# Five products instead of nine for the narrower segment of a two-batch unit

## What is computed

```python
def _attn_ref(q, k, v):            # (4, 8, 576, 64)
    scores = scale * np.matmul(q, k.transpose(0, 1, 3, 2))
    kth = np.partition(scores, -top_k, axis=-1)[..., -top_k:-top_k + 1]   # top_k = 32
    scores = np.where(scores >= kth, scores, -1000000000.0)
    scores = scores - np.max(scores, axis=-1, keepdims=True)
    attn = np.exp(scores)
    attn = attn / (np.sum(attn, axis=-1, keepdims=True) + 1e-09)
    return np.matmul(attn, v)
def _moe_ref(x, w_in, w_out):      # x (2304, 512), d_ff 2048
    h = x @ w_in
    return (h * (1.0 / (1.0 + np.exp(-h)))) @ w_out
def _moe2_ref(x, w1, w2, w3, w_out):   # d_ff 1024
    return (((x @ w1) * (x @ w2)) @ w3) @ w_out
```

## Time and profile before

| | |
|---|---|
| median of 3 runs | 1142.99 us (1142.81 to 1148.94) |
| the profiled execution | 1149.01 us |
| its span, first to last instruction | 1147.2 us |
| PE busy | 1065.4 us, 93% |
| DVE busy | 926.4 us, 81% |
| ACT busy | 773.1 us, 67% |
| POOL busy | 621.9 us, 54% |
| mean DMA rate | 271 GB/s |

### The profile page before, as it was taken

One profiled execution on the slowest core, in us unless ns is written; L12 is line 12 of the kernel. 1 busy time (PEld: TensorE's weight loads), 2 busy tenths in 40 slices (PEclk: granted clock), 3 DMA queues, 4 the chain that ended last, 5 costly groups with the idle time before them and its releaser, 6 DMA issues.

```text
span 1147.2 us, 24502 instructions
## 1 busy us (share of the span) xinstructions
PE 1065.4 (93%) x7968; PEld 995.4 (87%) x7968; DVE 926.4 (81%) x2042; ACT 773.1 (67%) x1921; POOL 621.9 (54%) x803
## 2 busy tenths in 40 slices
PE   2998478899999999999999999999999999999998
PEld 1554477799999999999999999999999999999997
DVE  5788877798888899998989999889899999991110
ACT  4577767777776677776767777767677777774221
POOL 4566768666664455566645555655455445543211
PEclk9999689999999999999999999999999999999999
DMA  9976769986997599779966996899569947963962
GB/s 283 329 270 240 262 234 311 312 262 217 338 354 263 172 326 357 243 245 355 360 210 217 330 343 199 269 356 352 198 224 321 327 145 259 343 212 120 332 242 92
DMA packets 129053, 310.42 MB, mean 271 GB/s; under 512 B 14240, under 2 KB 43936, under 8 KB 128928
## 3 DMA queue, kind: packets, MB, share of 16 engines
q1 hardware_dynamic: 110112, 275.30, 71.1%
q10 hardware_dynamic: 18816, 33.56, 8.3%
HBM read 263.19 MB, written 45.61 MB: 269 GB/s over the span
## 4 chain that ended last, share of the span: by engine, by line
PE 71%; DMA 10%; POOL 4%; DVE 4%; issue 4%; ACT 4%; ACTq 2%; SPq 1%; POOLq 0%; DVEq 0%
PE ps_x L934 7%; DMA win<-win_split 7%; PE ps_h L1002 6%; PE ps_h L1004 6%; PE ps_h L1003 6%; PE ps_s L905 5%; PE ps_h L964 5%; PE ps_h L965 4%; PE ps_h L966 4%; PE ps_y L986 4%; PE ps_y L988 4%; PE ps_y L987 4%; PE ps_t L920 4%; PE ps_y L1015 3%; PE ps_y L1016 3%
## 5 line engine op out<-in xcount | busy, mean ns | idle before, releaser
L809 DVE MAX8 top<-rest 128x8 f32<-128x576 f32 x432 | 309.8, 746 | 0.0
L620 POOL TENSOR_TENSOR g_lo<-gate,g_hi 128x256 fp32r<-128x256 f32 x216 | 160.0, 741 | 251.2 <-ACT g_hi L777 250.9
L811 DVE MATCH_REPLACE8 rest<-top,rest 128x576 f32<-128x576 f32 x288 | 212.9, 743 | 0.5
L964 PE MATMUL ps_h<-x_hi,win 128*128 128x256 f32 x576 | 167.1, 290 | 10.1 <-DMA win<-win_split 9.9
L1002 PE MATMUL ps_h<-x_hi,w_hi 128*128 128x256 f32 x576 | 166.1, 288 | 5.1 <-DVE x_lo L860 4.4
L608 POOL TENSOR_TENSOR pT<-p_raw,pT 128x640 fp32r<-128x640 f32 x72 | 113.4, 1575 | 102.5 <-ACT pT L737 102.5
L986 PE MATMUL ps_y<-g_hi,wout 128*128 128x256 f32 x576 | 165.8, 288 | 1.7 <-POOL g_lo L620 0.9
L1004 PE MATMUL ps_h<-x_hi,w_lo 128*128 128x256 f32 x576 | 162.7, 282 | 0.0
L1003 PE MATMUL ps_h<-x_lo,w_hi 128*128 128x256 f32 x576 | 162.7, 282 | 0.0
L965 PE MATMUL ps_h<-x_lo,win 128*128 128x256 f32 x576 | 162.5, 282 | 0.0
L966 PE MATMUL ps_h<-x_hi,win 128*128 128x256 f32 x576 | 162.3, 282 | 0.0
(11 more groups left out here) (73 smaller groups left out, 2793.8 us busy)
## 6 DMA issues: line engine op xcount, KB each, us to landing
win<-win_split SPq DMA_DIRECT2D x135, 512.0 KB, 6.3
wout<-wout_split SPq DMA_DIRECT2D x135, 512.0 KB, 4.8
wout<-w_dram SPq DMA_DIRECT2D x72, 512.0 KB, 3.9
v_split<-v_dram SPq DMA_DIRECT2D x64, 320.0 KB, 5.7
k_split<-k_dram SPq DMA_DIRECT2D x64, 288.0 KB, 5.7
v_dram<-v_split SPq DMA_DIRECT2D x32, 320.0 KB, 6.0
k_raw<-kT SPq DMA_DIRECT2D x64, 144.0 KB, 5.3
k_dram<-k_split SPq DMA_DIRECT2D x32, 288.0 KB, 6.8
```

What stands on the lines that cost most here:

```text
L809: nc.vector.max(best[:, 8 * n:8 * n + 8], sc if step == 0 else left).then_inc(topk_step, 1)
L811: nc.vector.match_replace(left, best[:, 8 * n:8 * n + 8], sc if step == 1 else left, BELOW_ALL).then_inc(topk_step, 1)
L964: nc.tensor.matmul(ps_h[:, f % 2, 0:UN], hi, xh, start=(c == 0), stop=False)
```

## The change

`beside(u)` names the narrower segment of a unit of two batches and its columns: segment 0 in unit 2, segment 1 in units 4 and 6. For it PV runs four products whose moving operand is two chunks of `pT` at once, the rounded one c and the remaining one c + 5, into two halves of the bank `ps_x`: columns c0 to c1, and the same 256 columns on. The fifth product is chunk 9 into the first half. XS adds the second half's rows of the rounded values to `x_raw` before its old addition; the second half's rows of the remaining values are not used (before, their product with the remaining probabilities was part of the sum). Since the second half of unit 2 lies where the tail was, `tail_at` puts the tail of that unit at column 384.

```diff
+def beside(u):
+    segs = segments(u)
+    if len(segs) < 2:
+        return None
+    n = 0 if segs[0][2] - segs[0][1] < P else 1
+    return n, segs[n][1], segs[n][2]
+
+def tail_at(u):
+    return UN + P if beside(u) and beside(u)[0] == 0 else UN
...
-        ps_tail = ps_x[0:D, UN:UN + P]
+        ps_halves = ps_x[:, :].rearrange("p (a n) -> p a n", a=2)
...
+        def tail(t):
+            at = tail_at(t // 2 // H)
+            return ps_x[0:D, at:at + P]
...
                 elif kind == "XS":
                     s = op[1]
                     dve.wait_ge(x_copied, s + 1)
                     mine = x_raw[hi_cols(s), (s // 2) % 2, :]
+                    if beside(s // H):
+                        _, c0, c1 = beside(s // H)
+                        part = x_raw[hi_cols(s), (s // 2) % 2, c0:c1]
+                        nc.vector.tensor_tensor(part, ps_x[hi_cols(s), UN + c0:UN + c1], part, ALU.add).then_inc(x_part, 1)
+                        dve.wait_ge(x_part, sum(1 for i in range(s + 1) if beside(i // H)))
                     nc.vector.tensor_tensor(mine, ps_x[lo_cols(s), 0:UN], mine, ALU.add).then_inc(x_summed, 1)
...
+                        if beside(s // H) == (seg, c0, c1):
+                            for c in range(KCH - 1):
+                                nc.tensor.matmul(ps_halves[:, :, c0:c1], v_split[:, e % NV, c, :], pT[:, c:c + KCH + 1:KCH, c0:c1],
+                                                 start=(c == 0), stop=False, skip_group_check=True)
+                            m = nc.tensor.matmul(ps_x[:, c0:c1], v_split[:, e % NV, KCH - 1, :], pT[:, 2 * KCH - 1, c0:c1],
+                                                 start=False, stop=True, skip_group_check=True)
+                            continue
```

More of the change, by code:

```diff
@@ L366, in build @@
         normed, transposed, p_rounded, p_split = sem("normed"), sem("transposed"), sem("p_rounded"), [sem("p_split0"), sem("p_split1")]
-        pv_ready, x_copied, x_summed, x_rounded, x_split = sem("pv_ready"), sem("x_copied"), sem("x_summed"), sem("x_rounded"), sem("x_split")
+        pv_ready, x_copied, x_summed, x_part, x_rounded, x_split = sem("pv_ready"), sem("x_copied"), sem("x_summed"), sem("x_part"), sem("x_rounded"), sem("x_split")
         h_ready, tanh_ready, g_ready, g_rounded, g_split = sem("h_ready"), sem("tanh_ready"), sem("g_ready"), sem("g_rounded"), sem("g_split")
@@ L730, in _ @@
                     if on_vector(t):
-                        nc.scalar.copy(pT[0:D, 2 * KCH - 1, cols], ps_tail)
+                        nc.scalar.copy(pT[0:D, 2 * KCH - 1, cols], tail(t))
                     else:
                         nc.scalar.copy(p_raw[:, lane, 0:KCH - 1], ps_t[:, :, :])
-                        nc.scalar.copy(p_raw[0:D, lane, KCH - 1], ps_tail)
-                        nc.scalar.copy(p_raw[D:P, lane, KCH - 1], ps_tail)
-                    nc.scalar.copy(pT[D:P, KCH - 1, cols], ps_tail)
+                        nc.scalar.copy(p_raw[0:D, lane, KCH - 1], tail(t))
+                        nc.scalar.copy(p_raw[D:P, lane, KCH - 1], tail(t))
+                    nc.scalar.copy(pT[D:P, KCH - 1, cols], tail(t))
                     nc.scalar.copy(pT[:, 0:KCH - 1, cols], ps_t[:, :, :]).then_inc(p_rounded, 1)
@@ L830, in _ @@
                                             ALU.subtract)
-                    nc.vector.tensor_tensor(pT[D:P, 2 * KCH - 1, cols], ps_tail, pT[D:P, KCH - 1, cols].bitcast(F32),
+                    nc.vector.tensor_tensor(pT[D:P, 2 * KCH - 1, cols], tail(t), pT[D:P, KCH - 1, cols].bitcast(F32),
                                             ALU.subtract).then_inc(p_split[t % 2], 1)
@@ L920, in _ @@
                         nc.tensor.transpose(ps_t[:, c, :], probs[:, t % 4, P * c:P * c + P], ident[:, :])
-                    nc.tensor.transpose(ps_tail, probs[:, t % 4, P * (KCH - 1):S],
+                    nc.tensor.transpose(tail(t), probs[:, t % 4, P * (KCH - 1):S],
                                         ident[:, :]).then_inc(transposed, 1)
```

## The result

| | before | changed |
|---|---|---|
| median of 20 runs | 1148.76 us | 1141.16 us |
| lowest to highest | 1142.81 to 1156.86 | 1134.75 to 1145.34 |
| profiled execution | 1149.01 | 1139.89 |
| its span | 1147.2 | 1138.0 |

The ratio is 0.9931 with a 95% interval of 0.9913 to 0.9950, that is 7.9 us saved (5.7 to 10.0); 8.3 was forecast. The time itself, 1141.16, lies 0.7 above the range's upper end of 1140.5, because the kernel before takes 1148.76 in the median of 20 runs and not the 1142.99 of the three from which I had subtracted.

The account below looks back on a forecast made before the run. TensorE (PE) was taken to bound all six two-batch stages. Products save 10.2 us, late loads take back 1.9, DVE's addition costs nothing: 8.3 us off the median 1142.99 gives 1134.7 us, range 1131.5 to 1140.5.

Parts of the forecast that it names:

- the base: Whole kernel: the time the saving is taken off, 1142.99 us, median of the runs shown, not the profiled 1149.01.
- The price of a product: PE's value products, 24 two-batch steps: weight load sets the pace, about 0.11 us each; four fewer per step save 10.2 us.
- The two runs of the moving operand: Double products on PE: operand in two runs, five chunks apart, costs nothing; at the dearest column price the sum is 7.2.
- DVE's addition hidden: XS on DVE: 6.6 us added, hidden by DVE's idle time and the 0.96 us before the next transposes.
- DVE at least 6 us busier: Sign in the profile after: DVE's busy time up by this much, with no new wait of the transposes for x_raw.
- What comes late next: First four steps of each two-batch stage: DMA loads of win come late and take back 1.9 us of the gain.
- landing is set by bytes, not by issue: Load of win in a first half's second step: queue full, so step 17's gain counts as lost.
- the bound of 354 to 361 GB/s: DMA in first halves: 353 to 357 GB/s needed to keep the whole gain; steps at 357 and 361 taken as its end.
- (c): Products on PE: columns set the price, so 9w for 9w saves nothing; about 1142.8 us; chance 0.07.
- (b): DVE becomes the bound or transposes wait for XS: 3.6 us saved, 1139.4 us; chance 0.07.
- (a): DMA engines take all the gain of the first halves: 5.1 us left, 1137.9 us; chance 0.17.
- (d): Slower: earlier loads meet k and v transfers, first halves fall to 320 GB/s; 8.1 us more, 1151 us; chance 0.05.

Follow-up runs that it names:

- e5: The kernel before, with each load of win bringing only the rounded half of the weights, 256 KB instead of 512 (H wrong); 1132.45 us, 0.9845 of before.
- e6: The changed kernel, with each load of win bringing only the rounded half of the weights (H wrong); 1124.62 us, 0.9775 of before.
- e3: The kernel before, nine products, but those of the narrower segment run over half their columns (part of the output left out); 1.0009 of before.
- e4: The changed kernel without XS's new addition and its wait (second half of the bank left out of the sum); 0.9935 of before.
- e7: The changed kernel with XS's new addition made four times, each waiting for the one ahead; 0.9981 of before.
- e8: The changed kernel with SP issuing all loads of win ahead of the wout load that waits for a later product; 0.9872 of before.
- e2: The changed kernel with the five products only in unit 4 (8 steps), units 2 and 6 keeping nine; 0.9993 of before.
- e1: The changed kernel with the five products only in units 2 and 6 (16 steps), unit 4 keeping nine; 0.9955 of before.
- after_again: The changed kernel measured once more, nothing altered; 1142.70 us, 0.9939 of before.
- v1_both_unit4: The changed kernel with both segments of unit 4 in five products and the tail at column 256 everywhere; 1140.09 us, 0.9894 of before.
- v1_again: A repeat measurement of the kernel with both segments of unit 4 in five products; 1139.61 us, 0.9909 of before.
- e10: The changed kernel with loads of win issued ahead of the waiting wout load from unit 1 on; 1132.28 us, 0.9854 of before.

## Why the prediction was right or wrong

**The step that failed: the base.** The forecast was a saving, 8.3 us, taken off a base, 1142.99 us. The saving was measured as 7.9, the base as 1148.76, 5.8 us higher. The sum was made against the profiled execution, 1149.01 - 8.3 = 1140.7 us, and 1141.16 was measured. I then took the 8.3 off 1142.99, the median of three runs, since the profiled one lay 6.0 above it. In the 20 runs of before, 1142.81 and 1142.99 are the two lowest, and 1149.01 is near the median of 1148.76. The profile was the typical execution and the two low runs were the luck. That there is a spread (14 us in 20 runs) could be seen in the data, as 6 us among three runs; the range should have been laid around both sums, 1134.7 and 1140.7, and would then have held the time.

**The price of a product** was right: four products less are 0.45, 0.42 and 0.45 us a step, 10.6 us in all by these rows and 10.2 by the stages of e5 and e6, with 10.2 forecast, and e3 shows that columns don't enter between 32 and 128. The rule of the Trainium skill that the forecast weighed ("TensorE: Matmul & The Clock Gate", section "Back-to-back issue gap") would have made it 0.24 us in all. The page gives that rule for an isolated matmul and says that it counts too little for few columns, since it leaves out the weight load; the forecast took it without this condition, and for this stream of loads and products the rows don't follow it.

**The two runs of the moving operand** cost nothing for 128 columns. For 256 the four products, with the passage to the fifth, take 0.52 us, where 0.47 was taken; the row is nonetheless 1.54 instead of the 1.56 worked out.

**DVE's addition hidden:** right, by e4 and e7, and both prices right to 0.01 us. The gap ahead of the transposes was the tighter cover, not DVE's share. A sign that I had named, DVE at least 6 us busier, did not come: the new additions are 5.8 us, but DVE as a whole was 4.5 us busier.

**What comes late next:** the place was right, the reason was not, and the size came out by luck. Step 17 kept nothing: 15.61 us before, 15.60 after, with the wait up from 0.72 to 1.16; the wait of step 33 rose from 1.22 to 1.83, that of step 49 fell from 2.07 to 1.64. But "landing is set by bytes, not by issue" does not hold, and with it falls the bound of 354 to 361 GB/s: e8 held 377 GB/s for 56.6 us, and a load issued 2 us sooner landed sooner. The trace of before had a sign of it, in a window of 5 us that I had not weighed:

```profile
330.00:335.00 5.00, 5.00 (x46) 5.00 (x45) 4.15 (x10) 3.22 (x8) 3.44 (x4) 1.00 1.04 416
```

For the size the twenty runs are the best measure: 7.9 us less the 5.2 of the last halves leave 2.7 us (0.5 to 4.8) for the first halves, where 10.2 - 1.9 - 5.1 = 3.2 were forecast. The profiles can't say it better, since the waits scatter. The first halves in us, of kernels that differ from before and changed in nothing meant to act there:

| | steps 16 to 19 | 32 to 35 | 48 to 51 |
|---|---|---|---|
| nine products | 60.2, 60.2, 65.3 | 59.1, 59.6, 63.9 | 60.7, 59.9, 60.4 |
| five products | 58.9, 61.9, 60.3, 60.3, 62.0, 60.8 | 58.0, 59.1, 58.9, 57.0 | 58.8, 60.4, 61.7, 59.2, 60.9, 61.8 |

(Nine: before, e2 or e1, e3. Five: changed, after_again, e4, e1 or e2, and outside unit 4 v1_both_unit4 and v1_again.) The means are 61.0 and 60.0; without e3, whose clock fell twice, the first is 59.9. So these profiles would give a first half anything from nothing to 1.0 us.

**The rivals.** (c) and (b) are ruled out by e3 and by e4. (a) named the right place, but its mechanism, full DMA engines, is no more than a part of it, and its size, 5.1 us, lies below the interval of 5.7 to 10.0; the smaller samples of e4 and after_again alone would allow it. (d) did not come in the median. In after_again a first half took 61.9 us, 1.7 more than in the kernel before, but with a fall of the clock, which (d) did not name.

## What to carry to other kernels

A matmul of 32 to 128 columns costs here 0.11 us whatever its width: put two moving operands behind one weight load before you narrow anything. When loads come late, read what the issuing engine was waiting for before you call the DMA engines full; a share of 1.00 did not mean that no more could be moved. Where an order of loads is changed, look at the whole span for what it does. And when a profiled execution and a median of three runs differ by more than the effect, carry both as bases of the range.

## What the runs showed of the hardware

**A wait can cost more than itself.** In e3, whose products are as long as those of before, step 18 takes 18.36 us and not 14.54. Behind a wait of 1.91 us for win the granted clock falls to 0.5, that is from 2.4 GHz to the other of its two levels, 1.2. Timeline of PE, then windows:

```profile
315.85 0.39 PE L966 MATMUL ps_h<-x_hi,win 128*128 128x256 f32 x1 [1.91 <-DMA win<-win_split]
```

```profile
310.00:315.00 5.00, 3.94 (x33) 3.74 (x31) 5.00 (x12) 4.98 (x15) 3.63 (x4) 1.00 1.02 352
315.00:320.00 5.00, 4.15 (x21) 4.15 (x21) 1.90 (x5) 1.23 (x3) 2.90 (x3) 0.61 1.04 413
320.00:325.00 5.00, 5.00 (x24) 5.00 (x24) 2.16 (x6) 0.36 (x1) 0.00 (x0) 0.50 0.57 183
325.00:330.00 5.00, 5.00 (x38) 4.98 (x38) 2.64 (x6) 2.68 (x7) 1.61 (x4) 0.86 0.58 212
```

PE is busy 5.00 of 5.00 us with 24 matmuls, where each window of the kernel before between 315 and 345 us has 44 to 46: busy time doesn't show it, the count and the clock do. Step 18 of e3 lost 3.8 us in all. In the seventeen profiles the clock fell so twelve times between 280 us and the end of the work, each time at the end of a wait for win of 1.79 to 2.71 us or within 2 us behind it; falls behind the last product are not counted. Five waits of 1.81 to 2.16 us, two of them in the kernel before, had no such fall. So the same wait comes with a fall in one execution and without one in another. Such falls are one source of the spread between executions. The ramp is another: the products of step 16 start between 281.1 and 291.6 us in these profiles. e10, where the longest wait for win is 0.7 us, spread over 0.7 us in four runs, the changed kernel over 10.6 in twenty. That the order of loads also calms the time is suggested by that and not shown, with so few runs.

**The rate.** Reads and writes together reached 377 GB/s over 56.6 us on this one core, 351 to 354 over the first halves where the loads are issued late. The Trainium skill, "HBM Reference", section "Specifications (TRN2)", gives about 358 GB/s as a core's share when both cores of a pair stream, and about 425 for a core that streams alone. With one core at work the trace agrees that 358 is no limit; how far above 377 this kernel could go no run here shows.
